# Taking GpSimd out of the first network's loop: a square on ScalarE, the denominator and g's low part on VectorE, y copied one slot earlier

## What is computed

```python
def _moe_ref(x, w_in, w_out, a, b):          # d_model 512, d_ff 2048
    h = x @ w_in
    h2 = h * h
    h3 = h2 * h
    P = a[0] + a[1] * h + a[2] * h2 + a[3] * h3
    Q = 1.0 + np.abs(b[0]) * np.abs(h) + np.abs(b[1]) * h2
    g = P / (Q + 1e-06)
    return g @ w_out

def _moe2_ref(x, w1, w2, w3, w_out):         # d_ff 1024
    return (((x @ w1) * (x @ w2)) @ w3) @ w_out
```

## Time and profile before

| | us |
|---|---|
| Time, median of 3 runs | 1227.45 |
| Lowest and highest | 1224.76, 1227.96 |
| Span of the profiled execution | 1225.8 |
| TensorE busy in it | 1165.7 |
| VectorE busy in it | 819.4 |
| ScalarE busy in it | 564.1 |
| GpSimd busy in it | 484.6 |

### The profile page before, as it was taken

How to read it: one execution, slowest core, us unless ns; L and a number is a source line. 1 busy time by engine, 2 the same in 40 slices (tenths; PEclk the granted TensorE clock), 3 DMA queues, 4 the chain that set the end, 5 groups by cost and what they waited for, 6 DMA issues and landing times.

```text
span 1225.8 us, 17014 instructions
## 1 busy us (share of the span) xinstructions
PE 1165.7 (95%) x5776; PEld 937.0 (76%) x5776; DVE 819.4 (67%) x1149; ACT 564.1 (46%) x1185; POOL 484.6 (40%) x416
## 2 busy tenths in 40 slices
PE   7988999899899899989989999999999999999998
PEld 6867777677678778768867887888888888888886
DVE  4389999789999999999998898881221212121211
ACT  4277888655555555555555555541212112121211
POOL 3535555456756757666665555540000000000000
PEclk9999999899999999999999999999999999999999
DMA  7968788311111121112110003521010101010000
GB/s 252 254 162 201 187 200 206 100 45 51 54 67 51 43 77 41 36 51 68 51 51 34 0 34 137 206 104 70 31 39 0 68 0 68 0 68 0 25 10 35
DMA packets 138162, 97.44 MB, mean 79 GB/s; under 512 B 88976, under 2 KB 117648, under 8 KB 137104
## 3 DMA queue, kind: packets, MB, share of 16 engines
q1 hardware_dynamic: 138128, 97.02, 26.5%
HBM read 65.54 MB, written 31.46 MB: 79 GB/s over the span
## 4 chain that ended last, share of the span: by engine, by line
PE 46%; DVE 28%; issue 5%; ACT 1%; POOL 1%; DVEq 0%; ACTq 0%; POOLq 0%
PE banks L1268 22%; PE banks L1283 10%; DVE nr L1172 9%; PE banks L1252 7%; PE banks L154 6%; DVE nr L1176 6%; DVE wq L1148 5%; DVE nr L1169 3%; DVE poly L1155 3%; POOL sq L979 1%; DVE x_lo L1135 1%; DVE poly L1158 0%; ACT rq L1054 0%; DVE y_sb L1143 0%; ACT habs L1044 0%
## 5 line engine op out<-in xcount | busy, mean ns | idle before, releaser
L154 PE MATMUL banks<-x_hi,weights 128*128 128x512 f32 x768 | 263.5, 404 | 17.1 <-DVE x_lo L1135 15.0
L1252 PE MATMUL banks<-g_hi,weights 128*128 128x512 f32 x768 | 259.3, 399 | 13.3 <-ACT y_sb L1069 9.6
L1268 PE MATMUL banks<-x_hi,weights 128*128 128x512 f32 x768 | 249.3, 396 | 0.0
L1209 DVE TENSOR_TENSOR nr<-habs,banks 128x512 f32<-128x512 f32 x48 | 33.0, 688 | 257.8 <-ACT habs L1101 257.8
L984 POOL TENSOR_TENSOR g_lo<-nr,g_hi 128x512 fp32r<-128x512 f32 x96 | 124.3, 1295 | 183.2 <-ACT g_hi L1062 183.2
L154 PEld LDWEIGHTS banks<-x_hi,weights 128*128 128x128 f32 x768 | 147.3, 192 | 56.2 <-DVE x_lo L1135 16.7
L1252 PEld LDWEIGHTS banks<-g_hi,weights 128*128 128x128 f32 x768 | 147.1, 192 | 53.2 <-ACT y_sb L1069 11.8
L979 POOL TENSOR_TENSOR sq<-wq,habs 128x512 f32<-128x512 f32 x96 | 159.7, 1663 | 41.4 <-DVE wq L1148 41.4
L1268 PEld LDWEIGHTS banks<-x_hi,weights 128*128 128x128 f32 x768 | 144.2, 188 | 34.8
L1054 ACT ACTIVATE rq<-sq,ln_bias 128x512 f32<-128x512 f32 x96 | 69.7, 726 | 208.3 <-POOL sq L979 208.3
L1172 DVE SCALAR_TENSOR_TENSOR nr<-nr,rq 128x512 f32<-128x512 f32 x96 | 157.8, 1644 | 3.3
(11 more groups left out here) (87 smaller groups left out, 1806.4 us busy)
## 6 DMA issues: line engine op xcount, KB each, us to landing
x_raw<-x_transposed_dram SPq DMA_DIRECT2D x12, 1024.0 KB, 5.4
weights<-second_mlp_weights_dram SPq DMA_DIRECT2D x8, 1536.0 KB, 6.6
second_mlp_weights_dram<-split SPq DMA_DIRECT2D x16, 512.0 KB, 3.0
qk_sb<-in_q SPq DMA_DIRECT2D x24, 256.0 KB, 3.3
qk_sb<-in_k SPq DMA_DIRECT2D x24, 256.0 KB
v_sb<-in_v SPq DMA_DIRECT2D x24, 256.0 KB, 3.0
x_transposed_dram<-y_sb SPq DMA_DIRECT2D x24, 256.0 KB, 3.3
x_transposed_dram<-y_sb SPq DMA_DIRECT2D x6, 1024.0 KB, 5.1
```

Source lines behind the costliest of these rows:

```text
L154: last = nc.tensor.matmul(bank[m % 4][:, :], slot[:, m, a, cols], x[:, c, :], start=c == 0 and n == 0, stop=c == KC - 1 and n == 2)
L1252: last = nc.tensor.matmul(bank[4 + c][:, :], slot[:, m, a, cols], g[:, m % G_BUFS, :], start=m == 0 and n == 0, stop=m == SLOTS - 1 and n ...
L1268: last = nc.tensor.matmul(bank[2 * (j % 2) + w][:, :], bslot[:, j, 2 + 2 * w + a, cols], x[:, c, :], start=c == 0 and n == 0, stop=c == KC ...
```

## The change

ScalarE now takes |h| with the scale -b0, so that habs holds |b0| |h|, and squares h into sq. VectorE makes s = |b1| h^2 + |b0| |h| in one instruction in place of w; GpSimd's multiplication goes. g_lo is made by VectorE, behind the two poly steps of the slot. The order on ScalarE becomes ln and exp of m+1, g_hi(m), h parts of m+2; y is copied in slot 0, at the end of the step on both engines. On GpSimd only the weight pieces (both halves in a row, behind g_lo of slots 2, 5, 8, 11) and the low parts of x remain.

```diff
-            def make_s(i, m):
-                u = m % 2
-                pool.wait_ge(w_ready, i * SLOTS + m + 1)
-                pool.tensor_tensor(out=sq[:, u, :], in0=wq[:, u, :], in1=habs[:, u, :], op=ALU.mult)\
-                    .then_inc(s_ready, 1)
...
             with pool.Fori(0, NBLK - 2) as i:
-                for m in range(1, SLOTS):
-                    step(i, m, pieces=True)
-                step(i + 1, 0)
...
+                for n in range(PIECES):
+
+                    pool.wait_ge(g_lo_ready, i * SLOTS + 3 * n + 3)
+                    piece_hi(i, n)
+                    piece_lo(i, n)
+                x_los(i + 1)
...
                 act.wait_ge(h_ready, i * SLOTS + m + 1)
-                nc.scalar.activation(habs[:, u, :], h[:, :], ACT.Abs).then_inc(habs_ready, 1)
+                nc.scalar.activation(habs[:, u, :], h[:, :], ACT.Abs, scale=ncoef[:, 4:5])
                 if not first:
                     act.wait_ge(g_ready, i * SLOTS + m - 1)
+                nc.scalar.activation(sq[:, u, :], h[:, :], ACT.Square).then_inc(h2_ready, 1)
...
-                if more:
-                    start_h(*nxt)
-                    ln_exp(*nxt)
+                if not (last and m == SLOTS - 1):
+                    ln_exp(*slot_after(i, m, 1))
+                g_his(i, m)
+                if not (last and m >= SLOTS - 2):
+                    start_h(*slot_after(i, m, 2))
                 if y_before is not None:
                     copy_y(y_before)
-                g_his(i, m)
...
-                step(i + 1, 0)
-                step(i + 1, 1, y_before=i)
+                step(i + 1, 0, y_before=i)
+                step(i + 1, 1)
...
-                nc.vector.tensor_scalar(wq[:, u, :], habs[:, u, :], bcoef[:, 1:2], bcoef[:, 0:1],
-                                        ALU.mult, ALU.add).then_inc(w_ready, 1)
+                dve.wait_ge(h2_ready, i * SLOTS + m + 1)
+                nc.vector.scalar_tensor_tensor(out=sq[:, u, :], in0=sq[:, u, :], scalar=bcoef[:, 1:2],
+                                               in1=habs[:, u, :], op0=ALU.mult, op1=ALU.add).then_inc(s_ready, 1)
...
+            def make_g_lo(i, m):
+                dve.wait_ge(g_hi_ready, i * SLOTS + m + 1)
+                nc.vector.tensor_tensor(out=g_lo[:, m % G_BUFS, :], in0=nr[:, m % 2, :],
+                                        in1=f32(g_hi[:, m % G_BUFS, :]), op=ALU.subtract).then_inc(g_lo_ready, 1)
...
-                    make_w(*nxt)
-                make_g(i, m, first)
-                if y_before is not None:
-                    copy_y(y_before)
+                    make_s(*slot_after(i, m, 1))
+                make_g(i, m)
                 if more:
-                    make_p(*nxt)
+                    make_p(*slot_after(i, m, 1))
+                make_g_lo(i, m)
+                if y_before is not None:
+                    copy_y(y_before)
```

More of the change, by code:

```diff
@@ L138, in __init__, with slot_after @@
         self.xt_stored = [sem(f"xt_stored{u}") for u in range(2)]
+def slot_after(i, m, n):
+    return i + (m + n) // SLOTS, (m + n) % SLOTS
 def x_chunk_ready(pe, sh, n, c):
@@ L872, in mlps @@
         habs = pl("habs", [P, 2, BLK])
-        wq = pl("wq", [P, 2, BLK])
         sq = pl("sq", [P, 2, BLK])
@@ L880, in mlps @@
         split = pl("split", [P, 2, BLK], F32R)
-        habs_ready, u_ready = sem("habs_ready"), sem("u_ready")
-        w_ready, s_ready, ln_ready, r0_ready = sem("w_ready"), sem("s_ready"), sem("ln_ready"), sem("r0_ready")
+        h2_ready, u_ready = sem("h2_ready"), sem("u_ready")
+        s_ready, ln_ready, r0_ready = sem("s_ready"), sem("ln_ready"), sem("r0_ready")
         t1_ready, t2_ready, e_ready = sem("t1_ready"), sem("t2_ready"), sem("e_ready")
@@ L997, in piece_lo @@
                                    op=ALU.subtract).then_inc(raw_split, 1)
[L999 to L1010, removed]
             pool.memset(ones[:, :], 1.0).then_inc(ones_ready, 1)
-            make_s(0, 0)
-            step(0, 0)
             pool.wait_ge(ones_ready, 1)
             with pool.Fori(0, NBLK - 2) as i:
-                for m in range(1, SLOTS):
-                    step(i, m, pieces=True)
-                step(i + 1, 0)
[L1020 to L1026, removed]
+                for n in range(PIECES):
[3 more added lines that the diff above has]
+                x_los(i + 1)
+            with pool.Fori(0, NBLK + 1) as i:
+                x_los(i + NBLK - 1)
         @block.scalar
@@ L1073, in step @@
                     x_his(i + 1, (h_ready, (i + 1) * SLOTS))
-                nxt = (i, m + 1) if m < SLOTS - 1 else (i + 1, 0)
-                more = not (last and m == SLOTS - 1)
-                if more:
-                    start_h(*nxt)
-                    ln_exp(*nxt)
+                if not (last and m == SLOTS - 1):
[3 more added lines that the diff above has]
+                    start_h(*slot_after(i, m, 2))
                 if y_before is not None:
                     copy_y(y_before)
-                g_his(i, m)
             start_h(0, 0, first=True)
@@ L1085, in _ @@
             ln_exp(0, 0)
-            ln_exp(0, 1)
-            g_his(0, 0)
+            step(0, 0)
             for u in range(2):
@@ L1143, in copy_y, with make_s @@
                     nc.vector.tensor_copy(y_sb[:, c, :], bank[4 + c][:, :]).then_inc(y_dve, 1)
-            def make_w(i, m):
-                u, g = m % 2, i * SLOTS + m
-                dve.wait_ge(habs_ready, g + 1)
-                nc.vector.tensor_scalar(wq[:, u, :], habs[:, u, :], bcoef[:, 1:2], bcoef[:, 0:1],
-                                        ALU.mult, ALU.add).then_inc(w_ready, 1)
+            def make_s(i, m):
+                u = m % 2
+                dve.wait_ge(h2_ready, i * SLOTS + m + 1)
+                nc.vector.scalar_tensor_tensor(out=sq[:, u, :], in0=sq[:, u, :], scalar=bcoef[:, 1:2],
+                                               in1=habs[:, u, :], op0=ALU.mult, op1=ALU.add).then_inc(s_ready, 1)
             def make_p(i, m):
@@ L1159, in make_p, with make_g @@
                                                in1=h[:, :], op0=ALU.add, op1=ALU.mult).then_inc(t2_ready, 1)
-            def make_g(i, m, first=False):
+            def make_g(i, m):
                 u, g = m % 2, i * SLOTS + m
                 dve.wait_ge(r0_ready, g + 1)
-                if not first:
-                    dve.wait_ge(g_lo_ready, g - 1)
                 nc.vector.scalar_tensor_tensor(out=nr[:, u, :], in0=sq[:, u, :], scalar=Q_ONE, in1=rq[:, u, :],
@@ L1177, in make_g, with step @@
                                                in1=nr[:, u, :], op0=ALU.add, op1=ALU.mult).then_inc(g_ready, 1)
-            def step(i, m, last=False, first=False, y_before=None):
+            def make_g_lo(i, m):
+                dve.wait_ge(g_hi_ready, i * SLOTS + m + 1)
+                nc.vector.tensor_tensor(out=g_lo[:, m % G_BUFS, :], in0=nr[:, m % 2, :],
+                                        in1=f32(g_hi[:, m % G_BUFS, :]), op=ALU.subtract).then_inc(g_lo_ready, 1)
+            def step(i, m, last=False, y_before=None):
                 if m == SLOTS - 2:
                     x_los(i + 1)
-                nxt = (i, m + 1) if m < SLOTS - 1 else (i + 1, 0)
                 more = not (last and m == SLOTS - 1)
                 if more:
-                    make_w(*nxt)
-                make_g(i, m, first)
+                    make_s(*slot_after(i, m, 1))
+                make_g(i, m)
+                if more:
+                    make_p(*slot_after(i, m, 1))
+                make_g_lo(i, m)
                 if y_before is not None:
                     copy_y(y_before)
-                if more:
-                    make_p(*nxt)
-            make_w(0, 0)
+            make_s(0, 0)
             make_p(0, 0)
[L1194 to L1197, removed]
+            step(0, 0)
+            step(0, 1)
             with dve.Fori(0, NBLK - 1) as i:
```

## The result

The changed kernel takes 1194.18 us, median of 4 runs (1191.05 to 1195.48), against 1226.7 for the kernel before in the same comparison: ratio 0.9733, 95% interval 0.9716 to 0.9751. That is 32.5 us less; 27.9 were forecast.

A forecast was written before the change was run, and what follows sets the result against it. VectorE, held up by GpSimd at SBUF, bounds the first network. Savings of 6.0 (block 0), 17.0 (blocks 1 to 3), 3.0 (block 4) and 1.9 (block 5) make 27.9 us: 1199.6 us, range 1193 to 1209.

The forecast's parts named there:

- rival (b): First network: TensorE is the bound at once, every block takes 90.05 us; 38.2 us saved, 1189 us; chance 14%.
- the wider one of 1189 to 1215: Whole kernel: the range in us that also takes in the rivals at 1189 us (14%) and 1215 us (15%).
- The port: VectorE's slot: two-SBUF-input steps and GpSimd exclude each other; without GpSimd's multiplication L1172 takes about 0.7 us, not 1.67.
- Rival (d): VectorE's slot: L1172 stays at 1.67 us with GpSimd gone; 51 us slower, 1278 us; chance 3%.
- The pieces: Blocks 0 to 3: GpSimd's weight pieces hold up s and L1169, 2.0 us a piece, 8 us a block.
- The copy of y: Slot 0: TensorE's 2.2 us wait and its slow clock go; VectorE waits some 1.2 us and copies for 1.35.
- The lead and the block's end: Slot 12: g_lo is ready 2.2 us before TensorE wants it, 0.8 in block 0; x_lo stalls 2.4 and 3.8.
- The rule for the block's end: Block's end: TensorE loses 4.6 us minus the lead of g_lo(12), but no less than 1.25, waiting for x_lo.
- slow clock: Behind the x_lo wait: TensorE loses 1.0 us in blocks 1 to 3 and 1.4 in block 0.
- The prediction's sentence that the clock is down after each such wait: Kernel before: after TensorE's x_lo and y waits 0.64 granted, or 12 matmuls take 4.61 or 4.44 us, not 2.75.
- The start: Block 0: starts with g_lo(0) 0.5 us later, because Square is in the way of ln.
- Rival (c): ScalarE: Square needs another table, two loads a slot; some 42 us longer, 1269 us; chance 3%.

The follow-up runs named there:

- the two subtractions: The changed kernel with one idle GpSimd subtraction in each slot without a piece: issued behind g_lo 1230.96 us, issued behind g 1192.47 us.

## Why the prediction was right, and where its sizes were off

The mechanism and the sign held. The size held by luck in part. The time, 1194.18, is just inside the 1193 to 1209 of the forecast, 32.5 us less where 27.9 were forecast. But the networks gained 36.0, which is nearer to the 38.2 of rival (b); with an attention as before the profiled run would have been 4.0 us shorter and outside that range, though inside the wider one of 1189 to 1215. Point by point.

**The port.** Right. The groups of VectorE's instructions in the first network of the changed kernel:

```profile
L1124 DVE SCALAR_TENSOR_TENSOR sq<-sq,bcoef,habs 128x512 f32<-128x512 f32 x96 | 81.4, 848 | 24.1 <-ACT sq L1023 23.8
L1141 DVE SCALAR_TENSOR_TENSOR nr<-sq,rq 128x512 f32<-128x512 f32 x96 | 80.7, 840 | 1.3 <-ACT rq L1034 1.3
L1144 DVE SCALAR_TENSOR_TENSOR nr<-nr,rq 128x512 f32<-128x512 f32 x96 | 76.2, 793 | 3.3
...
L1153 DVE TENSOR_TENSOR g_lo<-nr,g_hi 128x512 fp32r<-128x512 f32 x96 | 65.7, 685 | 0.7 <-ACT g_hi L1039 0.7
```

L1144 is the old L1172: 793 ns in the mean instead of 1644. s (L1124), whose bounds were 0.67 and 1.67, costs 0.66 start to start where nothing is beside it. An undisturbed slot is 4.76 us, 4.82 were forecast. Rival (d) fell with that, and the two subtractions showed it without any data dependence. What the forecast had not seen is that only the multiplication had to go. It priced VectorE's slot with g_lo in it and never asked what g_lo cost on GpSimd: nothing, by the run that puts it back.

**The pieces.** 2.0 us each were forecast. Timeline at one piece, GpSimd, then VectorE:

```profile
496.48 1.04 POOL L984 TENSOR_TENSOR split<-raw,ones 128x512 fp32r<-128x512 f32 x1 [13.79 <-DVE g_lo L1153]
497.60 1.62 POOL L989 TENSOR_TENSOR split<-raw,split 128x512 fp32r<-128x512 f32 x1
```

```profile
496.79 1.28 DVE L1124 SCALAR_TENSOR_TENSOR sq<-sq,bcoef,habs 128x512 f32<-128x512 f32 x1 [0.54 <-ACT sq L1023]
497.99 1.77 DVE L1141 SCALAR_TENSOR_TENSOR nr<-sq,rq 128x512 f32<-128x512 f32 x1
```

s is held up by 0.53, L1141 by 1.08: 1.6 us, at six of the sixteen pieces. At the other ten GpSimd begins while s is at work, s gets through in 0.74, and L1141 and L1144 are held up by 0.84 and 0.98: 1.8 us. So it is in block 0, where VectorE never waits and the pieces are 16.09 us apart, 1.8 more than three slots of 4.76.

**The copy of y.** The wait of TensorE went, as forecast, and the run with y in slot 1 priced it at 16.6 us. VectorE's own wait there was forecast at 1.2 us and isn't there, but for 2.5 us at the very last y: the copy follows g_lo at once.

```profile
526.11 0.68 DVE L1153 TENSOR_TENSOR g_lo<-nr,g_hi 128x512 fp32r<-128x512 f32 x1
526.81 1.37 DVE L1118 COPY y_sb<-banks 128x512 f32<-128x512 f32 x2
```

**The lead and the block's end.** This is the term that was mis-sized. The lead at slot 12 can be read from the trace. In block 2 g_lo(12) ends at 503.26, and TensorE begins with it at 506.47:

```profile
502.58 0.68 DVE L1153 TENSOR_TENSOR g_lo<-nr,g_hi 128x512 fp32r<-128x512 f32 x1
```

```profile
506.47 0.39 PE L1227 MATMUL banks<-g_hi,weights 128*128 128x512 f32 x1
```

That is 3.2 us in each of blocks 1 to 3, reckoned at 2.2, and in the same way 2.3 us in block 0, reckoned at 0.8: the slot was taken 0.06 too long and a piece 0.2 too dear, and a wait of 1.2 for y did not come. In block 4 it is 4.8 us at slot 12 and was so at slot 4 already. It stops growing there, because VectorE now waits for Square and through it for h; in blocks 1 to 3 the last piece takes 1.6 off it again.

The rule for the block's end, 4.6 less the lead but at least 1.25, did well. It gives 2.3 us over TensorE's 88.75 for block 0 and 1.4 for blocks 1 to 3; measured were 2.4 and 1.4. TensorE at the end of block 2:

```profile
509.81 0.50 PE L159 MATMUL banks<-x_hi,weights 128*128 128x512 f32 x1 [0.44 <-DVE x_lo L1110]
...
510.97 0.50 PE L159 MATMUL banks<-x_hi,weights 128*128 128x512 f32 x1 [0.19 <-POOL x_lo L977]
```

The second part of the mis-sizing is slow clock: 1.0 us in blocks 1 to 3 and 1.4 in block 0 were set down for it, and none came. With waits of 0.4 and 0.2 us (1.3 and 0.2 in block 0) in place of one of 3.8 the clock stays at 1.00. The prediction's sentence that the clock is down after each such wait was too strong for its own trace, too: behind the wait for y that ends at 452.54 us, of 1.5 us, 12 matmuls took 2.9 us there.

So blocks 1 to 3 took 90.2 us against 92.2 forecast: 6.0 us of the gap, half of it lead and half clock. Block 4 was forecast at 90.05 and came at 90.2. Block 0 was forecast at 94.0 and took 91.1, between these two matmuls:

```profile
258.59 0.50 PE L1227 MATMUL banks<-g_hi,weights 128*128 128x512 f32 x1 [1.92 <-DVE g_lo L1153]
...
349.72 0.39 PE L1227 MATMUL banks<-g_hi,weights 128*128 128x512 f32 x1
```

**The start.** g_lo(0) comes 10.55 us after the networks' start, 10.01 before: 0.5 later, as forecast. With that block 0 saved 8.8 us, 2.8 more than forecast. Block 5 saved 1.4 (1.9 forecast): the slow clock behind y is gone, but TensorE now waits 0.4 us for g_lo of the last slot.

**The sum.** Forecast 27.9 us for the networks, measured 36.0. Of these 8.1 us 6.0 are in blocks 1 to 3 and 2.8 in block 0, less 0.1 in block 4 and 0.5 in block 5, which makes 8.2. The medians show 32.5. Two profiles of the changed kernel have the attention 3.0 and 4.0 us longer than the profile before; for the runs without a profile that is not shown.

**ScalarE.** Rival (c) fell: the changed kernel has one table load of 1283 ns in all, as in the earlier trace rows, with Square in every slot. The Trainium skill (ScalarE: Activation LUTs, "Table sets: the hidden batching unit") says that cheap functions such as copy, identity and abs are in every set, and does not name Square there. What this run shows is that the one set loaded here has Square beside Ln and Exp; of other sets it shows nothing.

## What to carry to other kernels

In these runs a VectorE step of 128x512 fp32 with two SBUF operands and a GpSimd operation did not run side by side, nor did the tensor_scalar w, which reads one SBUF tensor; steps with one operand in PSUM and one in SBUF did. Before taking work off GpSimd, look which of VectorE's steps it lies beside, and first try issuing it beside those that read PSUM. A wait of TensorE next to a saturated engine can be only where the slack shows: give that engine its lead first, then move the transfer or copy. Here the other order lost 2.1 us of the network with the edit that was worth 16.6 afterwards.

## What had not been expected of the hardware

- Of two such operations the later one waits, but the next one of VectorE then waits for GpSimd in turn: an idle subtraction of 1.04 us cost VectorE 0.84 us a slot behind g_lo, and nothing when it was issued 2.0 us earlier.
- With both ready within 0.1 us GpSimd began first, and VectorE's operation bore the whole of it: four low parts took 3.6 us on two engines and 2.5 on VectorE alone.
- In the first network, waits of TensorE up to 1.4 us left the granted clock at 1.00 in every run, and each wait of 3.4 to 5.1 us came with a stretch at the lower level. Between 1.5 and 2.5 us both happened: of ten waits of 2.4 us for y, in the two kernels that copy it in slot 1 behind the changed s, four were followed by slow clock and six were not.
